# Two extra mask products ahead of each bias product in a gated linear-attention and mixture-of-experts kernel

## The reference, cut to what matters

```python
B, H, S, D = (4, 8, 768, 40)
for t in range(S):
    m_new = np.maximum(f_gate[:, :, t] + m, i_gate[:, :, t])
    f_stab = np.exp(f_gate[:, :, t] + m - m_new)
    i_stab = np.exp(i_gate[:, :, t] - m_new)
    C = f_stab[..., None, None] * C + i_stab[..., None, None] * np.einsum('bhd,bhe->bhde', vt, kt)
    n = f_stab[:, :, None] * n + i_stab[:, :, None] * kt
    h_tilde = np.einsum('bhde,bhe->bhd', C, qt)
    nq = np.einsum('bhd,bhd->bh', n, qt)[:, :, None]
    y[:, :, t] = sigmoid(o_gate) * h_tilde / np.maximum(np.abs(nq), 1.0)
x = y as 3072 tokens of 320 numbers
x = top-1 mixture of 8 experts (320 -> 1024 -> 320, ReLU), scaled per token
out = RMS norm, then gated feed-forward (320 -> 1536, SiLU, -> 320)
```

## Time and profile before

| | us |
|---|---|
| median of 3 runs | 1023.08 |
| lowest and highest run | 1017.5 and 1033.16 |
| span of the profiled execution | 1022.7 |
| stage 1, TensorE's first to last chunk product | 28.59 to about 297.5 |
| first experts' products | from about 319 |

### The profile page before, as it was taken

How to read it: one execution, slowest core, us unless ns; L and a number is a source line. 1 busy time by engine, 2 the same in 40 slices (tenths; PEclk the granted TensorE clock), 3 DMA queues, 4 the chain that set the end, 5 groups by cost and what they waited for, 6 DMA issues and landing times.

```text
span 1022.7 us, 18388 instructions
## 1 busy us (share of the span) xinstructions
PE 949.2 (93%) x6073; PEld 838.8 (82%) x6097; DVE 587.4 (57%) x1270; ACT 388.2 (38%) x676; POOL 122.2 (12%) x167
## 2 busy tenths in 40 slices
PE   2999999999945999999999959999999999999997
PEld 1677787877735999999999947888888888888887
DVE  6346575756765698787788824444544435345432
ACT  5112122222214767777777712333132223322222
POOL 6123233323320000000000011010010010100000
PEclk9667577776776999999999979999999999999999
DMA  6423222223029989999999810010010010100000
GB/s 209 106 61 98 76 68 86 80 73 93 14 85 271 266 262 266 263 275 288 244 288 301 249 40 27 1 51 2 1 51 0 0 51 0 51 0 0 27 1 26
DMA packets 78171, 111.24 MB, mean 109 GB/s; under 512 B 11840, under 2 KB 56128, under 8 KB 78128
## 3 DMA queue, kind: packets, MB, share of 16 engines
q1 hardware_dynamic: 74672, 101.51, 34.4%
q0 software_dynamic: 2304, 7.88, 2.2%
q10 hardware_dynamic: 1152, 1.31, 0.3%
HBM read 95.32 MB, written 15.35 MB: 108 GB/s over the span
## 4 chain that ended last, share of the span: by engine, by line
PE 91%; DVE 4%; DMA 2%; issue 2%; SPq 1%; ACT 1%; POOL 0%; ACTq 0%; DVEq 0%; POOLq 0%
PE bank L1331 40%; PE bank L1222 7%; PE bank L1406 4%; PE bank L1408 4%; PE bank L1407 4%; PE bank L1263 4%; PE bank L1355 4%; PE bank L1357 4%; PE bank L1356 4%; PE bank L1268 3%; PE bank L1276 2%; PE bank L1217 2%; PE bank L1230 2%; PE bank L1253 1%; PE bank L1237 1%
## 5 line engine op out<-in xcount | busy, mean ns | idle before, releaser
L1169 DVE TENSOR_TENSOR gated_lo<-gated,gated_hi 128x512 fp32r<-128x512 f32 x72 | 49.8, 692 | 184.8 <-ACT gated_hi L784 184.8
L779 ACT ACTIVATE sigm_sb<-bank 128x512 f32<-128x512 f32 x72 | 43.1, 599 | 253.2 <-PE bank L1331 253.2
L1331 PE MATMUL bank<-nT_hi,w_gv_hi 128*128 128x512 f32 x432 | 123.7, 395 | 2.6 <-DVE nT_lo L1156 2.6
L1331 PE MATMUL bank<-nT_lo,w_gv_hi 128*128 128x512 f32 x432 | 123.1, 394 | 0.0
L1331 PEld LDWEIGHTS bank<-nT_lo,w_gv_hi 128*128 128x128 f32 x432 | 81.3, 188 | 18.7
L1331 PEld LDWEIGHTS bank<-nT_hi,w_gv_hi 128*128 128x128 f32 x432 | 78.8, 188 | 16.9 <-DVE nT_lo L1156 2.8
L1331 PE MATMUL bank<-nT_hi,w_gv_lo 128*128 128x512 f32 x288 | 90.8, 396 | 0.0
L633 POOL DMA_INDIRECT c_rows<-y_by_slot,slot_idx x24 | 22.8, 948 | 566.5 <-issue 305.4
L1406 PE MATMUL bank<-w_out_hi,gated_hi 128*128 128x320 f32 x288 | 89.7, 311 | 0.0
L1408 PE MATMUL bank<-w_out_hi,gated_lo 128*128 128x320 f32 x288 | 89.1, 309 | 0.0
L1407 PE MATMUL bank<-w_out_lo,gated_hi 128*128 128x320 f32 x288 | 89.1, 309 | 0.0
(11 more groups left out here) (218 smaller groups left out, 1819.4 us busy)
## 6 DMA issues: line engine op xcount, KB each, us to landing
w_raw<-w SPq DMA_DIRECT2D x40, 640.0 KB, 6.7
w_raw<-w SPq DMA_DIRECT2D x40, 512.0 KB, 4.4
w_raw<-w SPq DMA_DIRECT2D x80, 128.0 KB, 4.8
kv_tok<-tok SPq DMA_DIRECT2D x24, 324.0 KB, 4.0
qk_sb<-qk SPq DMA_DIRECT2D x48, 160.0 KB
y_by_slot<-y_tile SPq DMA_DIRECT2D x12, 321.0 KB, 7.0
out_gate<-o_tok SPq DMA_DIRECT2D x4, 960.0 KB, 8.7
x_tile<-x_by_expert SPq DMA_DIRECT2D x12, 320.0 KB, 3.0
```

The source lines that it names most:

```text
L779: nc.scalar.activation(sigm_sb[f % 2][:], bank[2 * (f % 2)][:], ACT.Sigmoid).then_inc(sig_ready, 1)
L1169: dve.tensor_tensor(gated_lo[f % 4][:], gated[f % 2][:], gated_hi[f % 4][:].bitcast(F32), ALU.subtract).then_inc(hv_lo, 1)
L1331: m = mm(dst, w, x, start=(n == 0), stop=(n == len(terms) - 1))
```

## The change

Ahead of each 18-row bias product two products of the mask with the identity are issued into the same bank, each with start=True and stop=True, so that the next product, which also has start=True, overwrites them. They signal nothing. They stand behind the wait for `weights_ready`. All 24 chunks have two halves, so there are 2 x 2 x 24 = 96 more products of 128 rows by 512 columns in bf16.

```diff
                 for h in range(2):
                     wait(pe, weights_ready, 2 * i + h)
+                    for _ in range(2):
+                        mm(BIAS[:], ident16[:], maskT[:].rearrange("p a t -> p (a t)"), start=True, stop=True)
                     mm(BIAS[:], bias_key[p][:], bias_query[p][:].rearrange("r (a q) t -> r q a t", q=2)[:, h], start=True, stop=False)
                     mm(BIAS[:], ident16[:], maskT[:].rearrange("p a t -> p (a t)"), start=False, stop=True).then_inc(bias_ready, 1)
                     wait(pe, probs_ready, 2 * i + h - 1)
```

## The result

The changed kernel takes 1081.6 us (median of 4 runs, 1066.3 to 1085.7), the kernel before 1025.5 us beside it: the ratio is 1.051, 95% interval 1.045 to 1.056. I had forecast 981 us, in a range of 970 to 1003 us, and gave "slower" a chance of 0.12. The forecast is wrong, and on the wrong side.

The account below looks back on a forecast made before the run. TensorE's instructions at a clock that falls to half in stage 1 were taken as the bound: -64.1 us (clock stays high) + 19.4 + 3.4 (added products) = -41.3 us, from 1022.7 to 981 us, range 970 to 1003 us.

Parts of the forecast that it names:

- What bounds the kernel: Stage 1: TensorE waits for nobody, so its instructions set the time, 8.02 us a step at high clock, 14.45 at low.
- the front: First part of a stage 1 step, about 5 us at high clock, few full products; said to take the clock down.
- If the clock stays high: Stage 1 from 45 us on: the 144 us of low-clock time shrink by 64.1 us; given chance 0.70.
- rival 2: Stage 1: clock still falls in some steps; 999 us with a quarter of low time left, 1020 with half; chance 0.13.
- wrong at its root: Sign in stage 1: the clock falls in a step whose front holds six full mask products.
- expected 64.1 us of gain: Stage 1 from 45 us on: 144 us of low-clock time times 0.445, if the clock stays high.
- The price: Added products on TensorE in stage 1: 0.22 us each high, 0.42 low; 19.4 us plus 3.4 us at the beginning.
- Rival 3: Stage 1: the clock takes no notice of the added products; price 33 us, total 1055 us; chance 0.12.
- half of it left: Stage 1 with half the low-clock time remaining: gain 32 us, price 29 us, total 1020 us, no change.
- Rival 4: Stage 1: VectorE's chain from logits to the next step bounds the step; 1 us wait each, 1003 us; chance 0.05.
- The break-even: Stage 1: below some 65 us of low-clock time removed, worth 29 us, the change costs more than it brings.
- The 5.9 us: Stage 1: time TensorE was said to have waited on "issue" ahead of the scores, in 228 us.

Follow-up runs that it names:

- e1: Kernel before the change, with four extra mask products ahead of each bias product instead of two: 1011.0 us, ratio 0.984.
- e9: Kernel before the change, with the 18-row bias product issued four extra times ahead of each bias: 1134.4 us, ratio 1.107.
- e6: Kernel before, no added product, second half's bias and scores moved behind the increments: median 1085.1 us, 3 to 6% slower.
- e3: Kernel before the change, with the 18-row bias product issued two extra times ahead of each bias: 1081.0 us, ratio 1.055.
- e2: Kernel before, with four extra mask products a step in a row in attend, ahead of its weights-and-values products: 1040.6 us, ratio 1.015.
- e12: Kernel before, both halves' scores issued in turn behind the transposes, four extra mask products ahead of the first bias only: 974.3 us, ratio 0.949.
- e7: Kernel before, no added product, second bias and both halves' scores, issued in turn, placed behind the transposes: 1010.1 us.
- e11: Kernel before, both halves' scores issued in turn behind the transposes, two extra mask products ahead of the first bias only: 1022.0 us, ratio 0.984.
- e4: The changed kernel with a matrix of ones instead of the identity as weights of the extra products: 1075.4 and 1097.8 us.

## Why the prediction was wrong, point by point

**What bounds the kernel.** Right. Stage 1 lasts as long as TensorE's instructions, in the changed kernel too, and the clock decides. That the clock falls in the front is shown by the place of all 15 falls. That it is the front's poor fill that takes it down is borne out by e1 against e9, but for the type of the products; e6 shows that fill in a stretch isn't the whole rule.

**The step that failed: "If the clock stays high".** I took from the earlier trace rows which kind of product stands ahead of a fall and of a rise, and gave 0.70 to the case that four more full products a step suffice. No row said how many it takes. The place of one fall was shown. The piece around it (router's product, CARRY, first bias, first scores) gets only two of the four products; rival 2's argument came near to this, "the longest piece without a mask product (`logits`, CARRY) is not shortened", and was then outweighed. The fall at 81.3 us is exactly there, in a step of which the front holds six full mask products: the sign by which I said the forecast would be wrong at its root. The expected 64.1 us of gain didn't come: the low time grew from 144 to 205 us.

**The price was mis-sized.** Forecast 88 x 0.22 = 19.4 us plus 3.4 us. Measured 0.32 us high and 0.56 us low; the opening took 2.2 us longer (the third CARRY starts at 47.19 us and not at 44.98 us). The trace of before had the better number in the 0.32 us between a mask product and the scores, which I took for the upper bound, in favour of products in a long row. In the 293 us from 45 us on, 88 us high and 205 us low make 88/9.29 + 205/16.68 = 9.5 + 12.3 steps, so the price is 9.5 x 1.27 + 12.3 x 2.23 = 39.5 us. In the kernel before it was 96/8.02 + 144/14.45 = 12.0 + 10.0 steps; 2.3 more at the low clock, at 14.45 - 8.02 = 6.43 us each, make 15 us. Together 54 us, against 53 measured (293 - 240).

**Why more steps ran at the low clock.** A product added to a poor stretch lengthens it. If it doesn't lift the stretch far enough, it only puts more time between the full stretches, in which the clock comes back. e3 and e9 show this at its worst (0.61 and 0.58). e2 shows the other side: nearly as many products in the full stretch leave the low time at its 144 us. That the added length is all there is to the growth from 60% to 70% is argued, not shown.

**The rivals.** Rival 3's price, 33 us and 1055 us, was the nearest, but its reason is refuted: the clock does take notice (e1). What came was rival 2 in a form that I had not worked out: instead of a part of the low time left, more of it than before. I had bounded rival 2 at "half of it left", with no row that excluded a growth. The rule of the Trainium skill ("TensorE: Matmul & The Clock Gate", "Loop structure matters more than you think"), by which back-to-back matmuls stay at the high clock, isn't what these runs show: e9 is low 84% of the time from 45 to 396 us with TensorE busy without a gap. Rival 4 didn't occur here; VectorE is busy 6.78 us in a step of 9.29 us. Its beginning shows in e12, where VectorE is busy 7.32 of 8.22 us.

**The break-even** of 65 us of low time was too low for the same reason as the price. With steps of 9.29 and 16.68 us, 22 steps take the 240 us of before when 4.8 of them are low (4.8 x 16.68 + 17.2 x 9.29). So 5.2 of the 10 low steps, 5.2 x 14.45 = 75 us of low time, would have had to go.

**Two readings that were off.** The 5.9 us for which TensorE "waited" on issue are no wait either: all 48 weight loads of the mask product are in the trace of before and only 25 of its 48 matmuls, and the idle time stands where the first half's are missing. The conclusion, that nobody holds TensorE up, is only the stronger for it. And the front is shorter than the "about 5 us" of the prediction: 3.9 us from CARRY to the transposes (265.36 to 269.25), 4.7 us with the router's product ahead of it.

## What to carry to other kernels

A busy TensorE can be held at the high clock with products whose result is thrown away, but here it was nearly a matter of all or nothing: find the stretch in which the clock falls, fill it, and measure at twice the dose before judging; half a dose costs its full price and may lower the clock further. Take the price of such a product from where it will stand (between products of another type), not from a long row of them. Shorten the poor stretch as well: 40-row products on different rows of the array run side by side for the mere order in which they are issued. Alone, filling (e1, 1011 us) and shortening (e7, 1010 us) were worth 1 to 2%; together (e12, 974 us) 5%.

## What the runs showed of the hardware that I had not expected

- One more full product isn't one more step up: two a half gave 1081 us, three 1065 us, four 1011 us.
- In one and the same loop the clock can stay at either level: e11 ran 78 us high and then 155 us low, e6 34 us high and then 51 us low. In the kernel before and the changed one it came back within 28 us; what it takes to rise, these runs leave open.
- At the high clock a mask product costs 0.24 us in a row of four, 0.32 us in pairs between f32 products; an 18-row product of the neighbours' own type costs 0.235 us in a pair.
- Whether the weights are mostly zeros (identity) or ones made no difference to the clock that two executions could tell (e4).
